# Attention with window and block keys, routed experts, final layer on one core: where the sums of value blocks are made for the second to fifth pair of heads

## The reference

```
q, k, v: (2, 8, 768, 64); block, window = 32, 16; nb = 24
k_sum = k.reshape(B, H, nb, block, D).max(axis=3)
v_sum = v.reshape(B, H, nb, block, D).mean(axis=3)
scores_l = q @ k^T / 8, kept where |i - j| < window
scores_s = q @ k_sum^T / 8 + log(block)
a = softmax(concatenate([scores_l, scores_s], axis=-1))
x = a @ concatenate([v, v_sum], axis=2)
```

## Time and profile before

| | us |
|---|---|
| median of 3 runs | 581.48 (580.62 to 581.54) |
| the profiled execution | 577.67 |
| its span | 575.9 |
| PE busy | 554.9 (96%) |
| DVE busy | 400.8 (70%) |
| ACT busy | 291.1 (51%) |
| POOL busy | 128.4 (22%) |
| loads and stores | 74.42 MB in 63,450 packets |

### The profile page before, as it was taken

The page is one execution under the profiler, slowest core; times in us unless marked ns, Lnnn a source line. Parts: engine busy times, 40 slices in busy tenths (PEclk is TensorE's granted clock), DMA queues, the critical chain, the costliest instruction groups (busy, mean ns, idle before and its releaser), DMA issues.

```text
span 575.9 us, 12500 instructions
## 1 busy us (share of the span) xinstructions
PE 554.9 (96%) x4697; PEld 492.6 (86%) x4697; DVE 400.8 (70%) x1194; ACT 291.1 (51%) x600; POOL 128.4 (22%) x168
## 2 busy tenths in 40 slices
PE   6988999999999999999999999999999999999994
PEld 4666767798999999999999888988999988988983
DVE  4886657885767676663537688788887887777652
ACT  4777843424253433433345565556656665555541
POOL 5444400101001010103203153221112532222004
PEclk9999999999999999999999999999999999999998
DMA  8999310585445454546557322222222332100002
GB/s 282 272 250 252 93 46 1 177 291 176 160 162 201 170 197 149 174 158 237 199 195 203 90 75 73 74 73 75 73 74 73 114 126 58 34 0 1 1 1 109
DMA packets 63450, 74.42 MB, mean 129 GB/s; under 512 B 6496, under 2 KB 45408, under 8 KB 63392
## 3 DMA queue, kind: packets, MB, share of 16 engines
q1 hardware_dynamic: 61408, 67.35, 38.3%
q0 software_dynamic: 1984, 6.29, 3.2%
HBM read 67.34 MB, written 6.30 MB: 128 GB/s over the span
## 4 chain that ended last, share of the span: by engine, by line
PE 83%; DVE 6%; DMA 4%; ACT 2%; issue 2%; POOL 2%; SPq 0%; POOLq 0%; DVEq 0%; ACTq 0%
PE ps_h L1580 15%; PE ps_o L1598 14%; PE ps_o L1934 7%; PE ps_o L1935 7%; PE ps_o L1933 7%; PE ps_h L1933 7%; PE ps_h L1935 7%; PE ps_h L1934 7%; DMA v_blk<-in_v_heads 3%; PE ps_o L504 3%; PE ps_o L1629 2%; ACT prob L947 1%; POOL out L1914 1%; PE ps_s L1051 1%; PE ps_o L1557 1%
## 5 line engine op out<-in xcount | busy, mean ns | idle before, releaser
L1580 PE MATMUL ps_h<-x_e,raw_a 128*128 128x192 f32 x512 | 103.8, 338 | 0.0
L1598 PE MATMUL ps_o<-h_e,raw_b 128*128 128x192 f32 x512 | 94.0, 327 | 0.0
L1598 PEld LDWEIGHTS ps_o<-h_e,raw_b 128*128 128x128 f32 x512 | 84.6, 190 | 0.1
L1580 PEld LDWEIGHTS ps_h<-x_e,raw_a 128*128 128x128 f32 x512 | 82.2, 190 | 0.5
L1935 PE MATMUL ps_o<-b_hi,g_lo 128*128 128x512 f32 x192 | 75.9, 396 | 0.0
L1934 PE MATMUL ps_o<-b_lo,g_hi 128*128 128x512 f32 x192 | 75.8, 395 | 0.0
L1933 PE MATMUL ps_h<-y_hi,a_hi 128*128 128x384 f32 x220 | 74.4, 338 | 1.1 <-ACT h_sum L1761 1.1
L1933 PE MATMUL ps_o<-b_hi,g_hi 128*128 128x512 f32 x192 | 74.6, 389 | 0.0
L1935 PE MATMUL ps_h<-y_hi,a_lo 128*128 128x384 f32 x220 | 74.3, 338 | 0.0
L1934 PE MATMUL ps_h<-y_lo,a_hi 128*128 128x384 f32 x220 | 73.9, 336 | 0.0
L470 ACT ACTIVATE reach<-thr_mid,rest 128x256 bf16<-128x256 f32 x112 | 47.6, 496 | 42.2 <-DVE rest L234 42.2
(11 more groups left out here) (229 smaller groups left out, 1013.1 us busy)
## 6 DMA issues: line engine op xcount, KB each, us to landing
raw_a<-in_moe_w SPq DMA_DIRECT2D x32, 512.0 KB, 3.5
raw_b<-in_moe_w SPq DMA_DIRECT2D x32, 512.0 KB, 4.6
raw_a<-in_moe_w_in SPq DMA_DIRECT2D x30, 256.0 KB, 3.0
raw_b<-in_moe_w_out SPq DMA_DIRECT2D x15, 512.0 KB, 5.0
v_win<-in_v SPq DMA_DIRECT2D x8, 585.0 KB, 17.0
k_cols<-in_k SPq DMA_DIRECT2D x8, 384.0 KB, 15.5
q_cols<-in_q SPq DMA_DIRECT2D x8, 384.0 KB, 15.9
x_rows<-x_tok SPq DMA_DIRECT2D x8, 384.0 KB, 5.7
```

The source lines that it names most:

```text
L1580: ins = pe.matmul(ps_h[:, m % 2, 0:CAP], raw_a[r][:, kk, i * P:(i + 1) * P], x_e[e % 2][:, kk, :], start=kk == 0, stop=kk == KT - 1)
L1598: ins = pe.matmul(ps_y[:, d, 0:CAP], raw_b[r][:, i, d * P:(d + 1) * P], h_e[m % 2][:, :], start=m == 0 and d % 2 == 0, stop=m == MU - 1, s ...
```

## The change

The block sums of pairs 1 to 4 (the second to fifth) are made as the first pair's are, from the spans; their quarters are neither loaded nor halved, so that `v_blk` holds three pairs instead of seven. Pairs 5 to 7 keep the quarters. Values of pairs 1 to 4 are loaded in the place where their quarters were, ahead of the next pair's k and q. The block sums and their two copies move from the second group of the pair before to the pair's own first group. `keys(t + 2)` moves on VectorE from the first group, behind `out_rows`, to the second, ahead of it.

```
+                QUARTERS = 5
-                v_blk = asb("v_blk", [P, PAIRS - 1, 2, QUARTER * D])
+                v_blk = asb("v_blk", [P, PAIRS - QUARTERS, 2, QUARTER * D])
@@ sync
                     for t in range(1, PAIRS):
-                        load_quarters(t)
+                        if t < QUARTERS:
+                            load_v(t)
+                        else:
+                            load_quarters(t)
                         ...
                         if t + 1 < PAIRS:
                             load_k(t + 1)
                             load_q(t + 1)
-                        load_v(t)
+                        if t >= QUARTERS:
+                            load_v(t)
@@ gpsimd
-                        quarter_sums(pool, t)
+                        if t >= QUARTERS:
+                            quarter_sums(pool, t)
@@ vector
-                        if g == NG - 1 and t + 1 < PAIRS:
-                            means(dve, t + 1, 0, s_vm_first)
+                        if g == 0 and t >= 1:
+                            means(dve, t, 0, s_vm_first)
                         if G + 2 < GROUPS_A:
                             maxima(G + 2)
+                        if g == NG - 1 and t + 2 < PAIRS:
+                            keys(t + 2, t % 2)
                         out_rows(G)
-                        if g == 0 and t + 2 < PAIRS:
-                            keys(t + 2, t % 2)
@@ scalar
-                        if g == NG - 1 and t + 1 < PAIRS:
-                            means(act, t + 1, 1, s_vm_act)
+                        if g == 0 and t >= 1:
+                            means(act, t, 1, s_vm_act)
@@ tensor
-                    def first_block_sums():
-                        pe.wait_ge(s_v[0], 16)
-                        pe.wait_ge(s_bo, 4)
+                    def block_sums(t):
+                        pe.wait_ge(s_v[t % VS], 16 * (t // VS + 1))
+                        if t == 0:
+                            pe.wait_ge(s_bo, 4)
                         for j in range(NT):
                             blocks = block_of[0:WIN, BLOCK_COL - 2 * j:BLOCK_COL - 2 * j + TQ]
                             for e in range(2):
-                                ins = pe.matmul(sum_places(0)[e], blocks, v_win[0][0:WIN, j, e * D:(e + 1) * D],
-                                                start=j == 0, stop=j == NT - 1, skip_group_check=True)
+                                ins = pe.matmul(sum_places(t)[e], blocks, v_win[t % VS][0:WIN, j, e * D:(e + 1) * D],
+                                                start=t <= 1 and j == 0, stop=j == NT - 1, skip_group_check=True)
                         ins.then_inc(s_bs, 1)
-                    def block_sums(t):
+                    def sums_of_quarters(t):
                         ...
@@ tensor, the loop over groups
                         if G == 0:
                             turn(G, 1)
-                            first_block_sums()
+                            block_sums(t)
                             values(G)
-                        if g == NG - 1:
-                            if t >= 1:
-                                logits(t - 1, range(NG))
-                            if t + 1 < PAIRS:
-                                block_sums(t + 1)
+                        elif g == 0:
+                            block_sums(t) if t < QUARTERS else sums_of_quarters(t)
+                        elif g == NG - 1 and t >= 1:
+                            logits(t - 1, range(NG))
```

More of the change, by code:

```diff
@@ L645, in build @@
                 s_v = [sem(f"s_v{u}") for u in range(VS)]
-                s_vb = [sem(f"s_vb{t}") for t in range(1, PAIRS)]
+                s_vb = [sem(f"s_vb{t}") for t in range(QUARTERS, PAIRS)]
                 s_vr = sem("s_vr")
@@ L708, in quarter_sums @@
                 def quarter_sums(eng, t):
-                    eng.wait_ge(s_vb[t - 1], 16)
-                    tokens = v_blk[0:WIN, t - 1, :, :]
+                    eng.wait_ge(s_vb[t - QUARTERS], 16)
+                    tokens = v_blk[0:WIN, t - QUARTERS, :, :]
                     width = QUARTER * D
@@ L716, in quarter_sums @@
                                           ALU.add).then_inc(s_vr, 1)
-                        eng.wait_ge(s_vr, MEAN_ADDS * (t - 1) + i + 1)
+                        eng.wait_ge(s_vr, MEAN_ADDS * (t - QUARTERS) + i + 1)
                 def means(eng, t, e, done_sem):
@@ L754, in load_quarters @@
                     def load_quarters(t):
-                        sp.dma_start(v_blk[0:WIN, t - 1, :, :],
-                                     v_quarters[2 * t:2 * t + 2].rearrange("e r c -> r e c")).then_inc(s_vb[t - 1], 16)
+                        sp.dma_start(v_blk[0:WIN, t - QUARTERS, :, :],
+                                     v_quarters[2 * t:2 * t + 2].rearrange("e r c -> r e c")).then_inc(s_vb[t - QUARTERS], 16)
                     def store_rows(t):
@@ L1075, in first_block_sums @@
                             for e in range(2):
-                                ins = pe.matmul(sum_places(0)[e], blocks, v_win[0][0:WIN, j, e * D:(e + 1) * D],
-                                                start=j == 0, stop=j == NT - 1, skip_group_check=True)
+                                ins = pe.matmul(sum_places(t)[e], blocks, v_win[t % VS][0:WIN, j, e * D:(e + 1) * D],
+                                                start=t <= 1 and j == 0, stop=j == NT - 1, skip_group_check=True)
                         ins.then_inc(s_bs, 1)
-                    def block_sums(t):
-                        pe.wait_ge(s_vr, MEAN_ADDS * t)
+                    def sums_of_quarters(t):
+                        pe.wait_ge(s_vr, MEAN_ADDS * (t - QUARTERS + 1))
                         if t > HP:
                             pe.wait_ge(s_lc, 1)
-                        if t == 1:
+                        if t == QUARTERS:
                             pe.wait_ge(s_qo, 3)
@@ L1089, in block_sums @@
                             ins = pe.matmul(sum_places(t)[e], quarter_of[0:WIN, first:first + TQ],
-                                            v_blk[0:WIN, t - 1, e, 0:D], start=t == 1, stop=True,
+                                            v_blk[0:WIN, t - QUARTERS, e, 0:D], start=False, stop=True,
                                             skip_group_check=True)
```

## The result

The changed kernel takes 587.73 us (median of 4 runs, 586.19 to 590.5), the kernel before 581.48 us measured beside it (580.62 to 581.54): the ratio is 1.0116, 95% interval 1.0075 to 1.0158. It is slower by 6.2 us, where +5.1 was forecast.

What follows compares the result with a forecast made beforehand. PE's own work, not loads, was taken to bound the attention stage. Block sums +4.5, start -1.1, old fetch gaps -3.9 and new ones +5.6 gave +5.1 us on 581.48: 586.6 us, range 580.5 to 589.5.

Steps and rivals of the forecast that it cites:

- the chain of waits: Profile's list of waits in the attention stage, blaming a 19.8 us v_blk quarter load; the forecast disbelieved it.
- rival B: Attention stage: loads are the bound, so dropping four quarter loads makes it faster, -3.2 us, 578.3 us; chance 0.17.
- The fetch: PE's 256-instruction blocks arrive late behind attention loads: three old gaps go (-3.9 us), new ones come (+5.6 us).
- the time from block to block: On PE in the attention stage, one block's start until the next is usable: 7.7, 7.9 and 7.5 us.
- Rival A: All instruction fetches on PE hidden, so no gaps old or new: -0.5 us, 581.0 us; chance 0.14.
- a lighter load: Late in the attention stage the load backlog thins, shortening fetches: third gap 1.2 us, fourth 0.4 us.
- Block sums: On PE, sums from spans replace quarter sums in pairs 2 to 5: 4 x (1.40 - 0.27) = +4.5 us.
- The order: Moved sums, copies and keys in attention: -1.1 us at the start (bounds 0 and -1.5), zero elsewhere.
- The bad end: ScalarE's turned copies come late in the attention pairs: 0.3 us a pair, 2 us in all.
- The last x_tok: At the attention stage's end, its last x_tok was to come near 81.8 instead of 76.6 us.
- Rival D: ScalarE late 0.3 us a pair, fetches of 8.5 us: +8.0 at most, 589.5; forecast with C and D 0.69.
- the 3.8 us: Whole kernel: before's median lies 3.8 us above its profiled execution, a difference carried over to the forecast.

Runs made afterwards that it cites:

- loads_kept: The changed kernel with the four dropped quarter loads left in, read by nobody: 590.13 us, ratio 1.015 to the kernel before.
- before_spaced2: The kernel before with at most two attention loads in flight: 582.13 us, ratio 1.0013.
- sums_only: The changed kernel's sums from spans without those quarters, but with the kernel before's order: 585.48 us, ratio 1.006 to the kernel before.
- order_only: The changed kernel's order, but quarters loaded and halved for all seven pairs and no sums from spans: 582.42 us, ratio 1.0022 to the kernel before.
- before_spaced: The kernel before with at most three attention loads in flight (the spaced kernel before): 574.01 us, ratio 0.9873.
- before_spaced4: The kernel before with at most four attention loads in flight: 574.4 us, ratio 0.9871.
- after_spaced2: The changed kernel with at most two attention loads in flight: 580.17 us, ratio 0.9984 to the kernel before.
- order_spaced: The kernel before's sums in the changed kernel's order, with at most three loads in flight: 575.97 us, ratio 0.9905 to the kernel before.
- after_spaced: The changed kernel with at most three attention loads in flight: 581.37 us, ratio 1.0007 to the kernel before.

## Why the prediction was right, and where it was not

**The bound, and the chain of waits.** That PE, not the loads, bounds the stage held: fewer quarters did not speed it up, and rival B (the loads on the path, 578.3 us) fell. The chain's v_blk entry was a misattribution. The spaced kernel before still loads every quarter and is the fastest.

**The fetch.** That the gaps of rows 8 are late instruction blocks, that the denser blocks would make new ones, and that they would show at about 24, 32 and 40 us, was the centre of the forecast. They came at 25.1 to 27.6, 35.2 to 36.2 and 43.2 to 45.2. Their idle time with a fourth of 0.42 us at 18.85 is 6.0 us, forecast 5.6; three gaps of 3.9 went. That the two sums are alike is partly luck: the gaps were forecast as 1.9, 2.1 and 1.2 us and measured 2.49, 1.07 and 2.04. The step that was mis-sized is the time from block to block, forecast at 7.7, 7.9 and 7.5 us. It was 8.77, 8.60 and 9.00, which is 3.3 us more, and the slower work at half clock filled part of it, so that it did not show as a gap. Rival A, all fetches hidden, fell too. The Trainium skill's rule on "Runtime: NRT & Kernel Launch", section "Instruction fetch mechanics", that the fetch of the next block is mostly hidden, holds in the spaced kernels and not in the other ones; the measurement decides. What lay ahead of a packet was understood too simply. I expected a lighter load to thin the wait late in the stage; the packets' waits were 5.9, 5.75 and 6.4 us, no shorter than the 5.0 to 5.75 of before.

**What was missed: the clock.** No term of the sum had it: rows 3 and 9 have before's clock at 1.00, and the forecast took that for the changed kernel as well. In the profiled execution two stretches at half clock make PE's work 1.5 + 3.0 = 4.5 us longer, but not the kernel by as much. An estimate from the packets' times: the first stretch lies in the block from 27.62, whose successor began 1.6 us after its packet had landed, as the other late ones did (1.3 to 1.6); without the half clock PE would have stood still there 2.6 us in place of 1.07. The second lies in the block from 45.22. The packet of its successor landed at 50.57, so that this one could have begun at about 52.1, and it began at 54.08. So of the 4.5 us the clock cost about 2.0, if the packets had come at the same times, and the late blocks would have taken the rest in any case.

What makes the clock fall is not shown. It fell around a gap of 1.96 us in loads_kept and behind a wait of 1.80 us in before_spaced2; it stayed up behind gaps of 1.75 us in sums_only and 1.53 us in order_only. It also falls with no late block near: the first of two such stretches in before_spaced, after the attention stage, and the same work in before (windows with busy time, granted clock, DMA share and GB/s).

```profile
99.81:103.22 3.41, 3.41 (x27) 2.48 (x25) 2.49 (x16) 0.00 (x0) 1.15 (x1) 0.50 0.43 150
```

```profile
103.03:106.44 3.41, 3.28 (x50) 2.56 (x48) 2.68 (x18) 0.00 (x0) 1.24 (x1) 1.00 0.40 151
```

**Block sums**: the term 4 x (1.40 - 0.27) = +4.5 was 4 x (1.55 - 0.27) = +5.1. The first pair's sums of rows 6 write two banks and the new ones one, and a matmul holds PE 0.032 us instead of 0.029, inside the bounds given; whether the bank is the reason was not tested.

**The order**: forecast at -1.1 us from the start and zero elsewhere, it costs 1.6 to 2.0 where all quarters are kept. The gain at the start is there, less than I took: the value products of the fourth group start 0.45 us earlier than in before_spaced4 and 0.89 earlier than in before_spaced (27.15). Part of the 1.1 us was not the order's: the copy of keys(1), 0.76 us in rows 7, took 0.73 and 0.45 us in those two kernels, which have before's order. The bad end that I had named (ScalarE's turned copies late, 0.3 us a pair) is what happens, and most of all in the last pair. The timelines of ScalarE and PE in the last pair of the changed kernel:

```profile
82.25 0.82 ACT L730 ACTIVATE v_win<-ps_l 24x768 f32<-24x768 f32 x1
83.09 0.87 ACT L954 ACTIVATE prob<-ps_s,neg_max 128x120 f32<-128x120 f32 x3
83.84 0.50 ACT L962 ACTIVATE prob_t<-ps_t 120x384 f32<-120x384 f32 x1
```

```profile
84.39 0.57 PE L1115 MATMUL ps_o<-v_win,prob_t 120*64 120x65 f32 x12 [0.48 <-ACT prob_t L962]
```

The second half of the value products waits for a turned copy that stands behind the sums' copy and a run of exponentials. I had weighed the wait of the copy itself and not what its 0.8 us pushes back on its own engine.

**The sum, and why the median came out near.** Four traces give the stage's end with and without late blocks. The added work and the order are 80.89 - 75.44 = 5.45 us (forecast 4.5 - 1.1 = 3.4). Late blocks and the clock together cost the changed kernel 91.75 - 80.89 = 10.86 us and the kernel before 79.10 - 75.44 = 3.66 us. The difference is 7.2 us, some 5.2 of them without the clock (forecast 5.6 - 3.9 = 1.7). Together that is the measured 12.65, as it must be with the same four ends; the forecast's +5.1 was less than half of it. The last x_tok started at 88.74 us and not near 81.8. Rival D was nearest, as both of its causes came, but its sum leaves one out: +2.9 for fetches of 8.5 us is in it, the order's 2 us is not. With both it is +10.0 us, 591.5.

The median moved by only 6.2 us, because before's median lies 3.8 us above its profiled execution and the changed kernel's 2.8 below its own. The clock goes along with this. Of 53 runs of the kernel before beside the experiments, the ten with a mean clock of 0.995 or more have a median of 578.6 us, the 29 with 0.992 or less one of 582.4; the profiled execution, at 0.996, belongs to the first kind. So the 3.8 us, which I carried over as a constant, is mostly something that differs from run to run. That before's three gaps bring its half-clock stretches is a guess: no profile of before has one in its stage. For it speaks that nine of ten runs of after_spaced2 lie within 579.3 and 580.4, four of five of before_spaced within 573.5 and 574.4, and all of order_spaced within 0.7 us. Against it, after_spaced has no late block either, and its ten runs go from 579.53 at a mean clock of 0.997 to 583.63 at 0.990. That the forecast of 586.6 lies 1.1 us from the median is thus in good part luck: the loss in the stage was taken too small, and the distance between profile and median too large for the changed kernel. How far each run's distance is due to the clock alone was not taken apart.

## What to carry to other kernels

A gap in the middle of a run of equal instructions, marked "issue", deserves a look at the instruction queue's packets: if they lie as many instructions apart as a packet holds, the cure need not be in the engine's work; here it was in how many loads are in flight ahead of the fetch. Limiting those to three or four cost no bandwidth here and gained 1.3% (7.2 us), more than the 3.2 us that the best of the rivals gave the change; with two the loads became the bound of the kernel before. And before work is moved onto PE, count its instructions as well as its time. Where new gaps can arise, ask what the clock does behind them, and also whether PE would have waited anyway in that stretch, so that slow work costs nothing. And read before's median against its profile for what already varies.

## What the runs showed of the hardware that I had not expected

A 16 KB instruction packet began 5.0 to 6.4 us behind its block's first instruction while all loads were issued as early as buffers allow. In the kernel before with three or four loads in flight it was 0 to 2.2 us up to 50 us, and in the changed one with three up to 3.7, at nearly the same throughput (257 and 249 GB/s in the kernel before against 252 between 20 and 50 us). Two in flight gave no shorter waits in the kernel before (up to 2.6 us) and only 197 GB/s. After gaps of 2.49 and 2.04 us PE's granted clock was 0.50 for 3.41 and 6.83 us; after 1.07 us it stayed at 1.00. In before_spaced it was 0.50 for 3.41 us from 99.81, at work at which before had 1.00. Float32 products of 64 columns that alternate between the two halves of the output rows took 0.032 us a matmul, one of 128 columns onto all rows 0.11.
